# One cleared index transfer in the opening instead of six behind the first block, and GpSimd's first loop batch written out

## The chip, the cores and the metric

The kernel runs on one core of a Trainium2 chip. The metric is the device time of one execution in microseconds, median of the runs. TensorE (PE in the profile) multiplies matrices, VectorE (DVE) and ScalarE (ACT) work on rows of elements, GpSimd (POOL) does element work too and is the engine that issues the indirect transfers (gathers and scatters by a list of indices), and SyncE (SP) issues the plain transfers. Each engine runs its own instruction list in order. They meet only through semaphores: an instruction may raise one when it ends, and a later one on any engine may wait for a value.

## The reference: what is computed

Three layers in a row. The first is a linear attention over 4 batches, 8 heads, 768 steps, 48 dimensions:

```
for t in range(S):
    cur = einsum('bhd,bhe->bhde', u * k[t], v[t])
    y[t] = einsum('bhd,bhde->bhe', r[t], state + cur)
    state = w * state + einsum('bhd,bhe->bhde', k[t], v[t])
```

The second takes the 3072 rows of 384 values: `h = max(x@w1, x@w2, x@w3)` with 768 columns, then `h @ w_out`. The third is a mixture of 8 experts. Gate logits with a noise term choose the two best experts of each token, `relu(x @ w1[e]) @ w2[e]` is computed for the tokens of each expert, and the two results of a token are added with softmax weights.

## The kernel before

The attention goes in 24 chunks of 128 tokens, three of them to a block of 384 tokens, so there are 8 blocks. A block's chunks are computed while TensorE does the second layer of the block before: `period(i, b, half, attends, routes)` is one such stretch on each engine. In it TensorE does six groups of the second layer (`hidden`, three banks of PSUM each), puts the attention's products between them, and ends with three products by `w_out` (`x_product`, one for every 128 tokens). Each float32 product is made of three passes with split operands (lines 1445 to 1447, `three_pass`). Period 0 is written out on all engines, periods 1 to 6 are in a loop (`Fori(1, BATCH)`, two periods to a turn), and period 7 has no attention.

From period 1 on, each period also routes the block before it (`routes`): VectorE finds the two best experts of each token and the place of each token in its expert's list. GpSimd then writes six groups of 128 entries into `lists` in DRAM, by indirect transfers whose indices are in `row_i` (`put_entries`, L504: three groups of tokens, two choices each). An index above the bound writes nothing. The lists lie one period behind: in period i, GpSimd writes what VectorE prepared in period i-1 and completed at its end. So in period 1 there is nothing to write yet. GpSimd sets `entry` to 0 and all of `row_i` to SKIP (65535, above the bound) in the opening (L543, L544), and `put_entries(0)` in period 1 issues six transfers that write nothing but raise `listed` by 16 each. Those counts serve VectorE: `route_ranks(j)` waits until the entries that it is about to overwrite have been sent (`listed`), at 96 for the first block, at 96 more for each next one. SyncE and ScalarE wait for counts of the same semaphore near the end of the routing.

What the change and the prediction touch on the other engines: TensorE's `outputs` of the last chunk of a period (L1428, L1432) raises `y_mm`; VectorE waits for it before it adds `y_n` (L724, L726); TensorE's `turn_y` (L1440) waits for `y_n`; SyncE's load of the next values (L332) waits for `y_mm` too. At the end of period 0 this stands on TensorE as: `x_product(0, 0)`, `turn_y` of two chunks, `outputs` of chunk 5, `x_product(0, 1)`, `turn_y` of chunk 5, `x_product(0, 2)`, then period 1. ScalarE copies each `x_product` out of PSUM (`x_out`, L1225) and each turned y (L1163), and VectorE takes the low part of it (L732). The opening before period 0 has the same chain on chunk 2: `outputs`, `y_n`, `turn_y`, and then the small products `fold` (L1516).

Of the kernel before, what the change touches and what calls it, by code (L numbers as in the profile page):

```python
# [28 lines left out]
BATCH, HEADS, SEQ, HD = 4, 8, 768, 48  # L29
# [9 lines left out]
NTOK = BATCH * SEQ  # L39
# [5 lines left out]
BS = BT // P  # L45
NBLK = NTOK // BT
NE = 8
# [44 lines left out]
def build(nc, rT, kT, kN, vN, wcol, ucol, moe_w, gates, noise, ew1, ew2, out):  # L92
    ctx = ExitStack()
    with ctx:
        def sb(name, shape, dt=F32, where=None):
            return (where or ctx).enter_context(nc.sbuf_tensor(name, shape, dt))

        def sem(name):
            return ctx.enter_context(nc.semaphore(name))
# [3 lines left out]
        lists, blank = all_lists[0:NE * NTOK, :], all_lists[NE * NTOK:NE * NTOK + P, :]  # L103
# [79 lines left out]
        entry = sb("entry", [P, BS, 2, 4], I32, where=turn3)  # L183
        entry_f = sb("entry_f", [P, BS, 2, 4], where=turn3)
        row_f = sb("row_f", [P, BS, 2], where=turn3)
        row_i = sb("row_i", [P, 2, BS], I32, where=turn3)
# [57 lines left out]
        b_init = sem("b_init")  # L244
# [11 lines left out]
        entry_ok = sem("entry_ok")  # L256
        listed = sem("listed")
# [19 lines left out]
        block = ctx.enter_context(nc.Block())  # L277
        HALF = (slice(0, HB), slice(HB, P))

        def known(n, least):  # L280

            return isinstance(n, int) and n < least
# [10 lines left out]
        def _(sp):  # L293
# [99 lines left out]
            for q in range(NPE):  # L393
                if q == 3:
                    sp.wait_ge(ewh_ok, 1)
                    sp.wait_ge(ewl_ok, 1)
                src, at = (ew1, q * PIECE) if q * PIECE < W1P else (ew2, q * PIECE - W1P)
                sp.dma_start(e0_raw[q % 3][:, :], src[0, :, at:at + PIECE]).then_inc(e0_in[q % 3], 16)
                if q == 2:
                    sp.wait_ge(listed, 16 * 2 * BS * (NBLK - 1))  # L400
                    sp.wait_ge(x_stored, 16 * (NBLK - 2))
                    sp.wait_ge(x_clear, 16)
                    sp.dma_start(ent_e[:, :, :], lists[0:EARLY * ET, :].rearrange("(s p) w -> p s w", p=P)).then_inc(early_in, 16)
# [12 lines left out]
            sp.wait_ge(tile0_ok, 1)  # L416
            where = place(0, tile_0)
            sp.wait_ge(x_stored, 16 * NBLK)
            sp.wait_ge(listed, 16 * 2 * BS * (NBLK + 1))
            sp.wait_ge(xg_in, 32 * EARLY)  # L420
            load_entries(where, ent, entG_in)
            load_entries(where, ent3, entP_in)
# [20 lines left out]
        def _(pool):  # L443
# [35 lines left out]
            def own_values(b, cc):  # L479
                c, g = cc % BS, chunk(b, cc)  # L480
                pool.wait_ge(v_in[c], 16 * (2 * b + cc // BS + 1))
                pool.wait_ge(a_ok, g + 1)
                if not known(g, 1):
                    pool.wait_ge(yn_ok, g)
                pool.tensor_tensor(av[:, :].rearrange("j (n d) -> j n d", d=HD), v_sb[:, c, :, :].rearrange("j q (h d) -> j (q h) d", h=2),
                                   a_sb[:, :, :].rearrange("j q (h a) -> j (q h) a", a=1).to_broadcast([P, 2 * PAIRS, HD]),
                                   ALU.mult).then_inc(av_ok, 1)

            def prepare(b, cc):
                keys(b, cc)  # L490
                new_state(b, cc)

            def hidden_low(i, f):

                pool.wait_ge(hh_ok, F1T * i + f + 1)
                pool.tensor_tensor(hl[:, f, :], hmax[f % 3][:, :], hh[:, f, :].bitcast(F32), ALU.subtract).then_inc(hl_ok, 1)  # L496


            def put_entries(n, tokens=range(BS)):
                pool.wait_ge(entry_ok, n + 1)  # L500
                pool.sem_inc(passed, 1)
                for s in tokens:
                    for c in range(2):
                        pool.indirect_dma_start(  # L504
                            lists, bass.IndirectOffsetOnAxis(row_i[:, c, s:s + 1], 0),
                            entry[:, s, c, :], None, bounds_check=NE * NTOK - 1, oob_is_err=False).then_inc(listed, 16)

            def period(i, b, half, attends, routes):
                at = half * BS
                if attends:  # L510
                    prepare(b, at)
                if routes:
                    put_entries(i - 1)
                hidden_low(i, 0)
                hidden_low(i, 1)
                if attends:
                    own_values(b, at)
                    prepare(b, at + 1)
                hidden_low(i, 2)
                hidden_low(i, 3)  # L520
                if attends:
                    own_values(b, at + 1)
                    prepare(b, at + 2)
                hidden_low(i, 4)
                hidden_low(i, 5)
                if attends:
                    own_values(b, at + 2)
# [12 lines left out]
            pool.memset(empty[:, :, 0:1], 0).then_inc(b_init, 1)  # L540
            pool.memset(empty[:, :, 1:3], SKIP).then_inc(b_init, 1)
            pool.memset(empty[:, :, 3:4], 0).then_inc(b_init, 1)
            pool.memset(entry[:, :, :, :], 0).then_inc(b_init, 1)  # L543
            pool.memset(row_i[:, :, :], SKIP).then_inc(entry_ok, 1)  # L544
            pool.memset(pick[:, :, :, :], 0.0).then_inc(b_init, 1)
            pool.memset(zrow[:, :], 0.0).then_inc(b_init, 1)
# [2 lines left out]
            pool.iota(tok_id[:, :], [[P, BS]], base=0, channel_multiplier=1, allow_small_or_imprecise_dtypes=True).then_inc(const_ok, 1)  # L549
            pool.memset(carry[:, :], 0.0).then_inc(const_ok, 1)  # L550
            pool.iota(tile_f[:, 0, :], [[1, NTILE]], base=0, channel_multiplier=0, allow_small_or_imprecise_dtypes=True).then_inc(const_ok, 1)
            period(0, 0, 1, True, False)

            pool.wait_ge(lists_clear, 32)
            with pool.Fori(1, BATCH) as b:
                for half in range(2):
                    period(2 * b - 1 + half, b, half, True, True)

# [73 lines left out]
        def _(dve):  # L632
# [16 lines left out]
            for l in range(LEVELS):  # L649
                n = 1 << l  # L650
# [157 lines left out]
            def route_ranks(j, own, bank=7):  # L808

                rank = ps[bank][:, 0:BS * NE].rearrange("p (s e) -> p s e", s=BS)  # L810
                total = ps[bank][:, BS * NE:2 * BS * NE].rearrange("p (s e) -> p s e", s=BS)
                dve.wait_ge(rank_mm, j + 1)

                dve.wait_ge(listed, 16 * 2 * BS * (j + 1))
                for s in range(BS):
                    own(dve.tensor_tensor(POS[:, s, :], rank[:, s, :], carry[:, :], ALU.add))
                    own(dve.tensor_tensor(carry[:, :], carry[:, :], total[:, s, :], ALU.add))
                    own.settle()
                dve.sem_inc(rank_ok, 1)
# [42 lines left out]
            def period(i, b, half, attends, routes, first=False, final=False):  # L862
# [57 lines left out]
                if routes:  # L920
                    route_ranks(i - 1, own, 5 if final else 7)
# [227 lines left out]
        def _(act):  # L1149
# [43 lines left out]
            def hidden(i, f):  # L1193
                n = F1T * i + f

                act.wait_ge(h_mm, 3 * n + 1)
                if not known(n, 3):
                    act.wait_ge(hl_ok, n - 2)
                act.activation(hmax[f % 3][:, :], ps[0][:, 0:BT], ACT.Copy).then_inc(h0_ok, 1)

                act.wait_ge(hmax_ok, 2 * n + 2)
                if f == 0 and not known(i, 1):
                    act.wait_ge(x_mm, BS * i)
                act.activation(hh[:, f, :], hmax[f % 3][:, :], ACT.Copy).then_inc(hh_ok, 1)  # L1204
# [41 lines left out]
            def period(i, b, half, attends, routes, first=False, final=False):  # L1246
                at = half * BS
                for f in range(F1T):
                    hidden(i, f)
                    if attends and f in (0, 2, 4):  # L1250
                        fade(b, at + f // 2)
                    if routes and f == 0:
                        logs(i - 1)
                    if routes and f == 3:
                        gaps(i - 1)
                    if first and f < 3:
                        split_piece_high(3 + f)
                    if first and f == 1:
                        keep_gates()
                    if first and f == 2:  # L1260
                        split_fold_high(0)
                        split_fold_high(1)
                    if first and f in (3, 4):
                        split_wo_high(f - 3)
                    if final and f < NPE:
                        act.wait_ge(e0_in[f % 3], 16 * (f // 3 + 1))
                        split_high(0, f, 1, e0_raw[f % 3], f * PIECE)
                x_out(i, 0)
                if attends:
                    split_y_high(b, at, 3)  # L1270
                    split_y_high(b, at + 1, 4)
                x_out(i, 1)
                if attends:
                    split_y_high(b, at + 2, 7)
                if final:
                    turn_early(0)
                x_out(i, 2)
# [93 lines left out]
                early_high(1, q)  # L1371

            turn_rows(2)
            act.wait_ge(listed, 16 * 2 * BS * (NBLK + 1))
            act.wait_ge(plan_ok, 1)
            with act.Fori(0, NE // 2 - 1) as m:
                for par in range(2):
# [364 lines left out]
```

## Time and profile before

| | us |
|---|---|
| median of three runs (889.55 to 891.22) | 889.93 |
| the profiled execution's own time | 886.54 |
| its span, first to last instruction | 884.5 |
| TensorE busy | 869.8 |
| VectorE busy | 452.1 |
| GpSimd busy | 389.4 |
| ScalarE busy | 272.6 |

The span is what the trace covers; the execution's own time has 2.0 us around it. The runs that were timed took 3.4 us more than the profiled execution. TensorE is busy for 98% of the span, so the time is a sum of its work, of the few places where it waits and of those where its granted clock is below 1.00.

### The profile page before, as it was taken

The numbers are of one execution on the slowest core, as the hardware profiler recorded it, in microseconds if no ns is written. First come the engines' busy times: TensorE is split into PE (matmuls) and PEld (weight loads), VectorE is DVE, ScalarE is ACT, GpSimd is POOL, SyncE is SP. The second block draws the span as 40 slices with busy tenths as digits, with TensorE's granted clock in tenths as the row PEclk, the third lists the DMA queues.
The fourth block names the chain that finished last, engine by engine and source line by source line (L and its number), as shares of the span: only waits on it lengthen the run. The fifth ranks groups of instructions, "written<-read, shape, count | busy, mean of one in ns | idle before, by whom it ended". The sixth has DMA issues, their size and how long they took to land.

```text
span 884.5 us, 19490 instructions
## 1 busy us (share of the span) xinstructions
PE 869.8 (98%) x6540; PEld 846.3 (96%) x6541; DVE 452.1 (51%) x1100; ACT 272.6 (31%) x522; POOL 389.4 (44%) x380
## 2 busy tenths in 40 slices
PE   7999999999999999999999999999999999999997
PEld 5898999999999999999989999999999999999997
DVE  8762646547464655637473564353535435264322
ACT  4531323223141322225413343331414223143211
POOL 6344335344352534234443655453634435355543
PEclk9999999999999999999999999999999999999999
DMA  8894112222221221032115532624426252452222
GB/s 210 192 303 122 47 50 56 69 62 54 59 61 47 65 55 37 2 133 56 47 46 189 162 91 49 191 61 122 136 56 193 70 186 78 116 157 61 72 61 69
DMA packets 103763, 86.05 MB, mean 97 GB/s; under 512 B 60634, under 2 KB 93090, under 8 KB 103696
## 3 DMA queue, kind: packets, MB, share of 16 engines
q1 hardware_dynamic: 83152, 31.75, 15.2%
q0 software_dynamic: 12416, 26.28, 9.7%
q10 hardware_dynamic: 8128, 27.13, 9.4%
q8 instruction: 40, 0.66, 0.3%
q14 instruction: 27, 0.22, 0.1%
HBM read 70.46 MB, written 21.35 MB: 104 GB/s over the span
## 4 chain that ended last, share of the span: by engine, by line
PE 96%; issue 1%; POOL 1%; DVE 1%; another core or an unknown queue 1%; DMA 0%; ACT 0%; POOLq 0%; SPq 0%; DVEq 0%
PE ps L1445 28%; PE ps L1446 28%; PE ps L1447 28%; PE ps L1393 3%; PE ps L1432 2%; PE ps L1497 2%; PE ps L1428 2%; PE ps L1404 2%; PE ps L1419 1%; PE ps L1440 1%; POOL k_hat L466 1%; PE ps L1516 0%; DVE tables L652 0%; PE ps L1509 0%
## 5 line engine op out<-in xcount | busy, mean ns | idle before, releaser
L1445 PE MATMUL ps<-yh,wh 128*128 128x384 f32 x432 | 147.6, 342 | 0.7 <-ACT x_sb L1225 0.7
L1336 ACT ACTIVATE gh<-ps 128x384 fp32r<-128x384 f32 x136 | 67.0, 493 | 262.1 <-PE ps L1447 242.6
L1446 PE MATMUL ps<-xgl,w1h 128*128 128x384 f32 (+1 forms) x456 | 145.7, 320 | 1.5 <-issue 1.3
L1445 PE MATMUL ps<-xgh,w1h 128*128 128x384 f32 (+1 forms) x456 | 145.8, 320 | 0.5 <-issue 0.5
L1447 PE MATMUL ps<-xgh,w1l 128*128 128x384 f32 (+1 forms) x456 | 145.6, 319 | 0.3 <-issue 0.3
L1447 PE MATMUL ps<-yh,wl 128*128 128x384 f32 x432 | 144.6, 335 | 0.0
L1446 PE MATMUL ps<-yl,wh 128*128 128x384 f32 x432 | 144.5, 334 | 0.0
L1085 DVE SCALAR_TENSOR_TENSOR gl<-ps,gh 128x384 fp32r<-128x384 f32 x136 | 75.9, 558 | 129.6 <-ACT gh L1336 118.3
L1445 PE MATMUL ps<-w2h,gh 128*128 128x384 f32 x408 | 138.1, 338 | 0.0
L1446 PE MATMUL ps<-w2l,gh 128*128 128x384 f32 x408 | 136.5, 335 | 0.0
L1447 PE MATMUL ps<-w2h,gl 128*128 128x384 f32 x408 | 136.5, 335 | 0.0
L496 POOL TENSOR_TENSOR hl<-hmax,hh 128x384 fp32r<-128x384 f32 x48 | 51.5, 1073 | 129.6 <-ACT hh L1204 129.6
L590 POOL DMA_INDIRECT xg<-x_rows,ent x57 | 67.6, 1186 | 79.5 <-DMA ent<-lists 32.5
L760 DVE TENSOR_TENSOR hmax<-hmax,ps 128x384 f32<-128x384 f32 x96 | 53.2, 554 | 84.3 <-PE ps L1447 59.1
L504 POOL DMA_INDIRECT lists<-entry,row_i x54 | 54.0, 1000 | 85.1 <-DVEq L860 71.2
L617 POOL DMA_INDIRECT out<-yrow,ent x51 | 58.7, 1151 | 70.3 <-DVE yrow L1106 60.5
L1447 PEld LDWEIGHTS ps<-xgh,w1l 128*128 128x128 f32 x456 | 86.9, 191 | 1.6 <-issue 1.6
L1445 PEld LDWEIGHTS ps<-xgh,w1h 128*128 128x128 f32 x456 | 86.8, 190 | 1.2 <-issue 1.1
L1446 PEld LDWEIGHTS ps<-xgl,w1h 128*128 128x128 f32 x456 | 86.9, 191 | 0.3 <-issue 0.3
L1445 PEld LDWEIGHTS ps<-yh,wh 128*128 128x128 f32 x432 | 81.1, 188 | 3.0 <-issue 1.2
L608 POOL DMA_INDIRECT prev<-out,ent x51 | 52.1, 1022 | 70.0 <-issue 69.7
L1446 PEld LDWEIGHTS ps<-yl,wh 128*128 128x128 f32 x432 | 81.2, 188 | 0.0
(205 smaller groups left out, 1519.8 us busy)
## 6 DMA issues: line engine op xcount, KB each, us to landing
ew_raw<-ew ACTq DMA_DIRECT2D x28, 768.0 KB
v_sb<-vN SPq DMA_DIRECT2D x24, 192.0 KB, 2.7
out<-zrow SPq DMA_DIRECT2D x1, 4608.0 KB, 15.2
x_rows<-x_sb ACTq DMA_DIRECT2D x8, 576.0 KB
kn_sb<-kN SPq DMA_DIRECT2D x20, 192.0 KB, 3.6
k_raw<-kT SPq DMA_DIRECT2D x48, 72.0 KB, 1.9
wraw<-moe_w SPq DMA_DIRECT2D x6, 576.0 KB, 7.9
r_raw<-rT SPq DMA_DIRECT2D x44, 72.0 KB, 2.0
```

Source lines behind the costliest of these rows:

```text
L496: pool.tensor_tensor(hl[:, f, :], hmax[f % 3][:, :], hh[:, f, :].bitcast(F32), ALU.subtract).then_inc(hl_ok, 1)
L504: pool.indirect_dma_start(lists, bass.IndirectOffsetOnAxis(row_i[:, c, s:s + 1], 0), entry[:, s, c, :], None, bounds_check=NE * NTOK - 1, ...
L590: pool.indirect_dma_start(xg[:, s, :], None, x_rows, bass.IndirectOffsetOnAxis(ent[:, s, 0:1], 0), bounds_check=FAR, oob_is_err=False).the ...
L608: pool.indirect_dma_start(prev[:, s, :], None, out, bass.IndirectOffsetOnAxis(ent3[:, s, 2:3], 0), bounds_check=FAR, oob_is_err=False).the ...
L617: pool.indirect_dma_start(out, bass.IndirectOffsetOnAxis(ent2[:, s, 1:2], 0), yrow[:, s, :], None, bounds_check=FAR, oob_is_err=False).the ...
L760: dve.tensor_tensor(hmax[f % 3][:, :], hmax[f % 3][:, :], ps[1 + j][:, 0:BT], ALU.max).then_inc(hmax_ok, 1)
L1085: dve.scalar_tensor_tensor(gl[:, f, :], ps[f % 4][:, 0:T], 0.0, gh[:, f, :].bitcast(F32), ALU.max, ALU.subtract).then_inc(gl_ok, 1)
L1336: act.activation(gh[:, f, :], ps[f % 4][:, 0:T], ACT.Relu).then_inc(gh_ok, 1)
L1393: mm = pe.matmul(ps[bank + h][:, p * CH:(p + 1) * CH], k_hat[cc % 2][rows, p, :], q_hat[cc % 2][rows, p, :], start=True, stop=True)
L1445: pe.matmul(o, ah, bh, start=start, stop=False)
L1446: pe.matmul(o, ah, bl, start=False, stop=False)
L1447: return pe.matmul(o, al, bh, start=False, stop=stop)
```

## The change

A helper gives the count of `listed` after the entries of n blocks: `sets_put(n)` is 16 (one transfer in the opening) and 96 for each block. All waits for `listed` go by it. `entry` is cleared in one group only, and the opening ends with one indirect transfer of it with SKIP indices. Period 1 has `routes` False on GpSimd, so it issues no transfer. Periods 1 and 2 are written out ahead of the loop, which now starts at 2, and the wait for the cleared lists stands behind period 1. On the other engines only the values of the waits differ.

```diff
--- before.py
+++ after.py
@@ -277,6 +277,10 @@
         block = ctx.enter_context(nc.Block())
         HALF = (slice(0, HB), slice(HB, P))
 
+        def sets_put(n):
+
+            return 16 * (1 + 2 * BS * n)
+
         def known(n, least):
 
             return isinstance(n, int) and n < least
@@ -397,7 +401,7 @@
                 src, at = (ew1, q * PIECE) if q * PIECE < W1P else (ew2, q * PIECE - W1P)
                 sp.dma_start(e0_raw[q % 3][:, :], src[0, :, at:at + PIECE]).then_inc(e0_in[q % 3], 16)
                 if q == 2:
-                    sp.wait_ge(listed, 16 * 2 * BS * (NBLK - 1))
+                    sp.wait_ge(listed, sets_put(NBLK - 2))
                     sp.wait_ge(x_stored, 16 * (NBLK - 2))
                     sp.wait_ge(x_clear, 16)
                     sp.dma_start(ent_e[:, :, :], lists[0:EARLY * ET, :].rearrange("(s p) w -> p s w", p=P)).then_inc(early_in, 16)
@@ -416,7 +420,7 @@
             sp.wait_ge(tile0_ok, 1)
             where = place(0, tile_0)
             sp.wait_ge(x_stored, 16 * NBLK)
-            sp.wait_ge(listed, 16 * 2 * BS * (NBLK + 1))
+            sp.wait_ge(listed, sets_put(NBLK))
             sp.wait_ge(xg_in, 32 * EARLY)
             load_entries(where, ent, entG_in)
             load_entries(where, ent3, entP_in)
@@ -540,7 +544,7 @@
             pool.memset(empty[:, :, 0:1], 0).then_inc(b_init, 1)
             pool.memset(empty[:, :, 1:3], SKIP).then_inc(b_init, 1)
             pool.memset(empty[:, :, 3:4], 0).then_inc(b_init, 1)
-            pool.memset(entry[:, :, :, :], 0).then_inc(b_init, 1)
+            pool.memset(entry[:, 0, 0, :], 0).then_inc(b_init, 1)
             pool.memset(row_i[:, :, :], SKIP).then_inc(entry_ok, 1)
             pool.memset(pick[:, :, :, :], 0.0).then_inc(b_init, 1)
             pool.memset(zrow[:, :], 0.0).then_inc(b_init, 1)
@@ -549,10 +553,15 @@
             pool.iota(tok_id[:, :], [[P, BS]], base=0, channel_multiplier=1, allow_small_or_imprecise_dtypes=True).then_inc(const_ok, 1)
             pool.memset(carry[:, :], 0.0).then_inc(const_ok, 1)
             pool.iota(tile_f[:, 0, :], [[1, NTILE]], base=0, channel_multiplier=0, allow_small_or_imprecise_dtypes=True).then_inc(const_ok, 1)
+            pool.wait_ge(entry_ok, 1)
+            pool.wait_ge(b_init, 4)
+            pool.indirect_dma_start(lists, bass.IndirectOffsetOnAxis(row_i[:, 0, 0:1], 0), entry[:, 0, 0, :], None,
+                                    bounds_check=NE * NTOK - 1, oob_is_err=False).then_inc(listed, 16)
             period(0, 0, 1, True, False)
-
+            period(1, 1, 0, True, False)
             pool.wait_ge(lists_clear, 32)
-            with pool.Fori(1, BATCH) as b:
+            period(2, 1, 1, True, True)
+            with pool.Fori(2, BATCH) as b:
                 for half in range(2):
                     period(2 * b - 1 + half, b, half, True, True)
 
@@ -811,7 +820,7 @@
                 total = ps[bank][:, BS * NE:2 * BS * NE].rearrange("p (s e) -> p s e", s=BS)
                 dve.wait_ge(rank_mm, j + 1)
 
-                dve.wait_ge(listed, 16 * 2 * BS * (j + 1))
+                dve.wait_ge(listed, sets_put(j))
                 for s in range(BS):
                     own(dve.tensor_tensor(POS[:, s, :], rank[:, s, :], carry[:, :], ALU.add))
                     own(dve.tensor_tensor(carry[:, :], carry[:, :], total[:, s, :], ALU.add))
@@ -1371,7 +1380,7 @@
                 early_high(1, q)
 
             turn_rows(2)
-            act.wait_ge(listed, 16 * 2 * BS * (NBLK + 1))
+            act.wait_ge(listed, sets_put(NBLK))
             act.wait_ge(plan_ok, 1)
             with act.Fori(0, NE // 2 - 1) as m:
                 for par in range(2):
```

GpSimd's instruction list in the opening, before. The memsets and iotas end it, and the first work of period 0 follows:

```order
L549 IOTA tok_id 128x3
L550 MEMSET carry 128x8
L551 IOTA tile_f 128x26
L466 TENSOR_TENSOR k_hat<-k_raw,tables 128x512 [waits s_mm,rk_in0]
L476 TENSOR_TENSOR k_upd<-kn_sb,wu_nat 128x384 [waits u_mm,kn_in0]
```

The same place now:

```order
L553 IOTA tok_id 128x3
L554 MEMSET carry 128x8
L555 IOTA tile_f 128x26
L558 DMA lists<-entry,row_i 24576x4 [waits b_init,entry_ok]
L470 TENSOR_TENSOR k_hat<-k_raw,tables 128x512 [waits s_mm,rk_in0]
```

One indirect transfer has come between the last iota and period 0's first key product, with waits for GpSimd's own memsets.

GpSimd at the border of periods 0 and 1, before. `av` is the last work of period 0, and the loop starts at the branch:

```order
L485 TENSOR_TENSOR av<-v_sb,a_sb 128x384 [waits yn_ok,a_ok,v_in2]
L555 UNCONDITIONAL_BRANCH [waits lists_clear]
L555 ISA
L465 ISA [waits rk_in0]
L466 TENSOR_TENSOR k_hat<-k_raw,tables 128x512 [waits s_mm]
L472 REGISTER_ALU
L475 REGISTER_ALU [waits kn_in0]
L476 TENSOR_TENSOR k_upd<-kn_sb,wu_nat 128x384 [waits u_mm]
L500 REGISTER_ALU
L504 DMA lists<-entry,row_i 24576x4 [waits entry_ok]
L504 DMA lists<-entry,row_i 24576x4 x5
L495 ISA
```

The same place now:

```order
L489 TENSOR_TENSOR av<-v_sb,a_sb 128x384 [waits yn_ok,a_ok,v_in2]
L470 TENSOR_TENSOR k_hat<-k_raw,tables 128x512 [waits s_mm,rk_in0]
L480 TENSOR_TENSOR k_upd<-kn_sb,wu_nat 128x384 [waits u_mm,kn_in0]
L500 TENSOR_TENSOR hl<-hmax,hh 128x384 [waits hh_ok] x2
L489 TENSOR_TENSOR av<-v_sb,a_sb 128x384 [waits yn_ok,a_ok,v_in0]
```

The six transfers and the branch are gone from here. The branch into the loop now stands behind period 2.

## Rows read from the trace of the kernel before

**Rows 1.** The page: span and busy time of each engine.
```profile
span 884.5 us, 19490 instructions
PE 869.8 (98%) x6540; PEld 846.3 (96%) x6541; DVE 452.1 (51%) x1100; ACT 272.6 (31%) x522; POOL 389.4 (44%) x380
```

**Rows 2.** Waits of PE: waiter, releaser, us in total, times, longest.
```profile
PE ps L1440 <- DVE y_n L726: 2.0, 1, 2.0
```

**Rows 3.** Timeline of PE: start, us, instruction; in brackets idle time before and releaser.
```profile
73.82 0.39 PE L1432 MATMUL ps<-v_sb,scores 128*64 128x48 f32 x8
...
77.33 0.34 PE L1447 MATMUL ps<-woh,hl 128*128 128x400 f32 x1
79.64 0.52 PE L1440 MATMUL ps<-ident,y_n 128*128 128x128 f32 x3 [1.97 <-DVE y_n L726]
...
84.10 0.54 PE L1445 MATMUL ps<-woh,hh 128*128 128x400 f32 x1
```

**Rows 4.** Timelines of DVE, SP and ACT, the same stretch.
```profile
78.87 0.46 DVE L724 TENSOR_TENSOR y_n<-ps,av 128x288 f32<-128x288 f32 x1 [5.07 <-remote]
...
78.86 0.39 SPq L332 DMA_DIRECT2D v_sb<-vN  x1
...
81.83 0.51 ACT L1225 ACTIVATE x_sb<-ps 128x400 f32<-128x400 f32 x1 [8.70 <-remote]
```

**Rows 5.** Windows: us, busy time of each engine, PEclk, DMA share, GB/s.
```profile
82.00:84.00 2.00, 2.00 (x7) 1.97 (x7) 1.25 (x3) 0.72 (x2) 0.00 (x0) 0.50 0.00 0
```

**Rows 6.** Timeline of POOL around the six transfers.
```profile
73.12 1.16 POOL L504 DMA_INDIRECT lists<-entry,row_i  x1 [0.17 <-issue]
...
79.69 0.97 POOL L504 DMA_INDIRECT lists<-entry,row_i  x1 [0.30 <-issue]
91.13 1.00 POOL L496 TENSOR_TENSOR hl<-hmax,hh 128x384 fp32r<-128x384 f32 x1 [10.46 <-ACT hh L1204]
```

**Rows 7.** Timelines around period 2's batch: POOL, then PE, then ACT, then DVE.
```profile
137.04 1.01 POOL L504 DMA_INDIRECT lists<-entry,row_i  x1 [9.08 <-DVEq L860]
...
143.48 0.97 POOL L504 DMA_INDIRECT lists<-entry,row_i  x1 [0.30 <-issue]
...
141.40 0.33 PE L1447 MATMUL ps<-yh,wl 128*128 128x384 f32 x1
...
145.68 0.49 ACT L1199 ACTIVATE hmax<-ps 128x384 f32<-128x384 f32 x1 [1.54 <-PE ps L1447]
...
140.30 0.56 DVE L760 TENSOR_TENSOR hmax<-hmax,ps 128x384 f32<-128x384 f32 x1 [1.10 <-issue]
```

**Rows 8.** Period 1's end: `outputs` in the chain, `y_n` in DVE's timeline.
```profile
128.22 0.22 PE ps L1432 x8
...
128.49 0.46 DVE L724 TENSOR_TENSOR y_n<-ps,av 128x288 f32<-128x288 f32 x1
```

**Rows 9.** The chain: third attention products of a period, first ones of the next.
```profile
66.89 1.09 PE ps L1393 x16
94.39 1.09 PE ps L1393 x16
...
274.52 1.09 PE ps L1393 x16
298.50 1.09 PE ps L1393 x16
```

**Rows 10.** The opening: timelines of POOL, DVE and PE.
```profile
31.54 1.38 POOL L466 TENSOR_TENSOR k_hat<-k_raw,tables 128x512 f32<-128x512 f32 x1 [6.28 <-DMA r_raw<-rT]
...
26.46 0.46 DVE L724 TENSOR_TENSOR y_n<-ps,av 128x288 f32<-128x288 f32 x1 [0.56 <-PE ps L1432]
26.84 0.25 DVE L726 TENSOR_TENSOR y_n<-ps,av 128x96 f32<-128x96 f32 x1
...
27.57 0.55 PE L1440 MATMUL ps<-ident,y_n 128*128 128x128 f32 x3
```

**Rows 11.** DMA queues in 74 to 76 us: packets, MB, share.
```profile
q8 instruction: 1, 0.02, 4.4%
```

## The prediction

> **What bounds the kernel now.** I read the page first. TensorE is busy 869.8 of 884.5 us, over 98% [rows 1]. So an edit on GpSimd is worth only what it changes in TensorE's idle time or clock. The list of TensorE's waits is the next view. Past the start its longest entry is 2.0 us, once, at L1440 behind VectorE's y_n [rows 2]. That one is to be followed, because it stands beside the six transfers that the change takes away.
>
> The timeline of TensorE shows it. `outputs` of chunk 5 ends at 73.82 + 0.39 = 74.21, `x_product(0, 1)` ends at 77.67, and then TensorE stands until 79.64 because `turn_y` needs y_n [rows 3]. VectorE began that y_n at 78.87, after 5.07 us idle, though its inputs were long made: the product ended at 74.21, 4.66 us earlier. The profile puts the wait down to "remote", that is, to nothing it knows. SyncE's load of values, which waits for the same semaphore, starts at 78.86. ScalarE's copy of `x_product(0, 1)` starts at 81.83, 4.16 us after that product's end [rows 4]. Three engines that wait for a signal of TensorE all got it over 4 us late. At the end of period 1 the same y_n starts at 128.49, 0.05 us behind its product [rows 8].
>
> What lies beside it is GpSimd's batch: six transfers from 73.12 to 80.66, 0.97 us each and 0.30 between them [rows 6]. The last late signal comes 81.83 - 80.66 = 1.17 us behind the last transfer. Period 2's batch has the same mark: its last transfer ends at 144.45, TensorE's first-bank product (L1447) ends at 141.73, and ScalarE, waiting for it at the end, starts at 145.68, which is 1.23 us behind the batch [rows 7]. There TensorE does not stop, since nothing it needs soon hangs on that signal. So I read it thus: while GpSimd issues a batch of indirect transfers, TensorE's signals can reach the others some 4 us late, and only at the end of period 0 does TensorE itself need the answer at once.
>
> The stand has a sequel. In 82 to 84 us the granted clock is 0.50, the lower of its two levels (1.2 GHz), and the matmul at 84.10 takes 0.54 us where the one at 77.33 takes 0.34 [rows 3, 5]. TensorE had stood for 1.97 us shortly before the fall.
>
> **The change part by part.** *Six transfers leave period 1.* GpSimd gets 7.54 us back (73.12 to 80.66), none of it on the path: its next work waited for ScalarE until 91.13 anyway, 10.46 us of idle [rows 6]. What counts is the late signal. With no batch there, I take y_mm to arrive at 74.2 as in period 1. Then y_n is done by 75.0, 2.7 us before TensorE asks for it, so the 1.97 us go, and with them the fall of the clock. The size is taken from the chain instead of from those two pieces: from the third attention products of period 0 to the first ones of period 1 is 94.39 - 66.89 = 27.50 us. The same stretch between periods 4 and 5, with the same instructions on TensorE and no wait, is 298.50 - 274.52 = 23.98 [rows 9]. The difference is 3.52 us. The pieces agree: 1.97 of it is the stand, and the 1.55 left are what some 3.1 us at half the clock lose, of which the 2 us of [rows 5] are a part. What is late next is nothing: that other stretch has no stop at all.
>
> *One transfer enters the opening.* It starts where GpSimd fell idle, at 31.54 - 6.28 = 25.26, and the engine has nothing else to do until 31.54, when its data arrives [rows 10]. Its 0.97 to 1.16 us [rows 6] are hidden five times over in the 6.28 us of idle. Queued behind it is only that key product. But its mark on TensorE's signals has to be bounded. In the opening the chain is tight: y_mm for chunk 2 gives y_n at 26.46, done at 27.09, and TensorE starts `turn_y` at 27.57 without a wait [rows 10], so the slack is 0.48 us. From below: no delay, as at first in period 2's batch, which began at 137.04: VectorE's L760, which waits for TensorE, had its signal by 140.30 [rows 7]. The cost is 0. By the mark of the batches: the transfer ends at about 25.3 + 1.16 = 26.46, release comes 1.17 us later, at 27.63, y_n starts 1.17 us late, and beyond the slack TensorE loses 0.7 us. From above: the longest delay seen, 4.66 us, less the slack, 4.2 us. I take 0.4, between the first two, since a single transfer is nearest to the start of a batch.
>
> *The count waits.* `route_ranks(0)` waits for 16 in place of 96 and finds it long reached. Later waits are for the same transfers as before, each count being 80 lower. *Written-out periods 1 and 2.* The same work on GpSimd without register arithmetic; a code block more or less to load is hidden in idle stretches like the 10.46 us before 91.13. The wait for the cleared lists moves behind period 1, over 50 us after it was met. *The smaller memset* is 0.12 us on an idle engine. Each of these is 0.
>
> **Sum.** -3.5 + 0.4 = -3.1 us. On the profiled execution that is 886.54 - 3.1 = 883.4. The timed runs are at 889.93, 3.4 above it, and I carry the same difference over: 889.93 - 3.1 = 886.8 us.
>
> The Trainium skill has a rule against this reading. The page "SBUF — State Buffer", section "Who interferes with whom", says that transfers never contend with a compute engine, and that TensorE and ScalarE wait for no one. By that rule the batch couldn't have held TensorE up and the sum would be 0 (889.9 us). The trace agrees that TensorE's own reads went on, since the matmuls run on through the batch; that its signals came 4 us late is in rows 4, and the rule says nothing of signals.
>
> **The rivals.** *A: the late signal has another cause, and it stays.* One candidate is loading of code: TensorE comes to its loop here, and in 74 to 76 us one packet of code was loaded [rows 11]. The others are the many loads that SyncE issues at this time, and the profiler itself, in which case the timed runs never had the stand. For it: period 2's late signal cost nothing, so there is one costly case only. Against it: both late cases lie by a batch and end 1.2 us behind it, and TensorE's instructions did go on through 74 to 77.67. The time is then that of before, 889.9 us, or 890.3 with the opening's 0.4. The page "Runtime: NRT & Kernel Launch", section "Instruction fetch mechanics", states that a taken branch out of the loaded window stalls for a fetch; by that rule the stand would belong to the loop and the time would be the 889.9 of this rival.
>
> *B: slower, the delay moves into the opening.* There SyncE's loads are dense too. The point that decides is y_mm of chunk 2: each microsecond that it is held beyond 0.48 is one that TensorE stands. If it is held as long as at 74.21, that is 4.2 us of stand, and a stand of that length brings the half clock with it, 1.5 us as above: 5.7 - 3.5 = +2.2, 892.1 us. It breaks even at a delay of 2.5 us with a fall of the clock (2.0 + 1.5). Against it: one transfer instead of six, ended before the late part of any batch seen.
>
> *C: half of it.* The stand is shorter but not gone, because VectorE or ScalarE is late for its own reasons, and the clock still falls: -1.6 us, 888.3.
>
> **How the numbers follow.** My forecast has 0.68, A 0.18, B 0.07, C 0.07. About 0.2% (1.8 us) is what a measurement of this kernel can tell from no change. The forecast lies at 886.4 (nothing lost in the opening) to 887.1 (0.7 lost), and with the spread of the runs (0.4 below and 1.3 above their median) at 885.5 to 888.1. It gives nearly all of "faster", 0.70 with a share of C; "same" has A and most of C, 0.22; "slower" is B, 0.08. For the range I reach from 885.4 over C and A to 890.5, which leaves out B and the tails.
>
> **What would show it.** Right: TensorE's 2.0 us behind y_n (L726 before, L735 now) is gone from the list of waits; y_n of chunk 5 starts near 74.3 and has no "remote" before it; the granted clock is 1.00 in 82 to 84; the stretch between the products is near 24.0 us; in the opening y_n starts by 27.6. Wrong: y_n stays late with no transfer of GpSimd near it (A), or TensorE stands at the `turn_y` of 27.57 (B), or the profile shows the gain and the timed runs don't (A, the profiler).

## The result and the profile after

The changed kernel takes 883.77 us (median of 6 runs, 882.47 to 885.45), and the kernel before 890.39 (6 runs of the same comparison, 889.02 to 891.48). The ratio is 0.9925, its interval 0.9913 to 0.9937, so the change saves 6.6 us. I had forecast 886.8, some 3.1 saved. The direction was right, the size half of what came, and the time lies below my range.

The profiled execution of the changed kernel took 883.59 us. This is its page.

```profile
span 881.8 us, 19454 instructions
PE   867.1 (98%) x6540; PEld 844.5 (96%) x6541; DVE 451.3 (51%) x1100; ACT 272.1 (31%) x522; POOL 383.4 (43%) x375
```

TensorE is busy 2.7 us less than in [rows 1] with the same 6540 instructions: part of its work ran at a higher clock. GpSimd has five instructions fewer. TensorE's list of waits (columns as in [rows 2]) begins so:

```profile
PE ps L1582 <- POOLq L462: 4.1, 1, 4.1
PE ps L1402 <- POOL k_hat L470: 1.8, 2, 1.1
PE ps L1456 <- issue: 1.5, 2, 1.0
PE ps L1455 <- issue: 1.0, 1, 1.0
PE ps L1454 <- ACT x_sb L1234: 0.7, 1, 0.7
```

The 2.0 us behind y_n of [rows 2] are gone, and no entry of this list stands in that stretch: the first is at the program's start, the waits for `k_hat` are at 10 and 16 us, the others behind 180 us. The timelines of VectorE, ScalarE and GpSimd answer to [rows 4] and [rows 6]:

```profile
74.29 0.46 DVE L733 TENSOR_TENSOR y_n<-ps,av 128x288 f32<-128x288 f32 x1 [0.45 <-PE ps L1441]
...
77.75 0.50 ACT L1234 ACTIVATE x_sb<-ps 128x400 f32<-128x400 f32 x1 [4.58 <-PE ps L1456]
...
87.39 1.01 POOL L500 TENSOR_TENSOR hl<-hmax,hh 128x384 fp32r<-128x384 f32 x1 [14.41 <-ACT hh L1213]
```

y_n starts at 74.29, where [rows 4] had 78.87, and ScalarE copies `x_product(0, 1)` at 77.75 in place of 81.83. Both have TensorE as their releaser again, not "remote". The windows (columns as in [rows 5]) and the chain of the stretch of [rows 9] show what TensorE makes of it:

```profile
80.00:84.00 4.00, 4.00 (x25) 4.00 (x24) 0.87 (x4) 0.99 (x2) 0.00 (x0) 1.00 0.49 158
```

```profile
66.93 1.09 PE ps L1402 x16
90.66 1.09 PE ps L1402 x16
```

The clock stays at 1.00, and the stretch takes 90.66 - 66.93 = 23.73 us, where [rows 9] had 27.50. In the opening, timelines of GpSimd, VectorE and TensorE answer to [rows 10]:

```profile
25.45 1.50 POOL L558 DMA_INDIRECT lists<-entry,row_i  x1 [0.19 <-issue]
...
26.93 0.46 DVE L733 TENSOR_TENSOR y_n<-ps,av 128x288 f32<-128x288 f32 x1 [1.00 <-PE ps L1441]
...
27.61 0.55 PE L1449 MATMUL ps<-ident,y_n 128*128 128x128 f32 x3
```

y_n starts 0.47 us later than before, at the very end of the transfer (25.45 + 1.50 = 26.95). It stays within the slack: TensorE has `turn_y` at 27.61, against 27.57.

The two profiled executions differ by 886.54 - 883.59 = 2.95 us, close to my sum of 3.1, but by luck: the stretch alone gave 27.50 - 23.73 = 3.77, the opening cost next to nothing, and about 1 us of the lead was lost again in small pieces behind the stretch (3.7 us at 90.66, 2.7 between the spans). The timed runs differ by 6.6. That was the riddle the experiments had to solve.

### The profile page after: what moved, and what is told of

The parts are those of the page before. It is cut to its first block, busy times and chain, and to the rows that moved or that the text cites. A ratio compares the mean times of both kernels' runs of the same rounds, so it can differ in the third digit from the quotient of the medians.

```text
span 881.8 us, 19454 instructions
## 1 busy us (share of the span) xinstructions
PE 867.1 (98%) x6540; PEld 844.5 (96%) x6541; DVE 451.3 (51%) x1100; ACT 272.1 (31%) x522; POOL 383.4 (43%) x375
## 4 chain that ended last, share of the span: by engine, by line
PE 97%; issue 1%; POOL 1%; DVE 1%; DMA 0%; POOLq 0%; ACT 0%; SPq 0%; DVEq 0%
PE ps L1454 28%; PE ps L1455 28%; PE ps L1456 28%; PE ps L1402 3%; PE ps L1441 2%; PE ps L1506 2%; PE ps L1437 2%; PE ps L1413 2%; PE ps L1428 1%; PE ps L1449 1%; POOL k_hat L470 1%; PE ps L1525 0%; DVE tables L661 0%; DMA u_sb<-ucol 0%; PE ps L1518 0%
## 5 line engine op out<-in xcount | busy, mean ns | idle before, releaser
L1454 PEld LDWEIGHTS ps<-yh,wh 128*128 128x128 f32 x432 | 81.1, 188 | 3.2 <-issue 1.4
L508 POOL DMA_INDIRECT lists<-entry,row_i x48 | 47.2, 983 | 83.4 <-DVEq L869 71.2
```

What stands on the lines that cost most here:

```text
L508: pool.indirect_dma_start(lists, bass.IndirectOffsetOnAxis(row_i[:, c, s:s + 1], 0), entry[:, s, c, :], None, bounds_check=NE * NTOK - 1, ...
L1454: pe.matmul(o, ah, bh, start=start, stop=False)
```

## The experiments

My theory at this point: GpSimd's batch of indirect transfers delays TensorE's signals, and taking it away is the whole gain. Rival: the written-out periods, the code that they load or the loads of SyncE are behind the delay. The first four kernels ran on one chip, with 23 runs of the kernel before, median 890.12 (886.26 to 891.75).

**The kernel before, profiled again.** No edit.

> The kernel before, unchanged, run again for its spread and for a second trace. Theory 1 (the late signal at the end of period 0 costs more in a typical execution than in the one first traced): y_n of chunk 5 again starts over 4 us behind its product, and the stretch between the third attention products of period 0 and the first of period 1 is 27.5 us or more, up to 30.6, since the timed runs lost 6.6 us against the changed kernel and the two traces 2.7. Theory 2 (the first trace was simply a fast execution, and a typical one has more stops or half-clock stretches elsewhere): that stretch is again about 27.5 us, and some 3 us more are lost behind it, most likely at 435 to 460 us.

Measured: 889.97 us (12 runs, 887.96 to 892.25), ratio 1.0 (0.9987 to 1.0012). Its profiled execution took 890.85, 4.3 us more than the one I had predicted from. The same stretch of it, in TensorE's waits, then in the timelines of VectorE and GpSimd:

```profile
PE ps L1440 <- DVE y_n L726: 4.9, 1, 4.9
```

```profile
81.59 0.46 DVE L724 TENSOR_TENSOR y_n<-ps,av 128x288 f32<-128x288 f32 x1 [8.01 <-remote]
...
72.90 1.16 POOL L504 DMA_INDIRECT lists<-entry,row_i  x1 [0.18 <-issue]
...
79.47 0.97 POOL L504 DMA_INDIRECT lists<-entry,row_i  x1 [0.30 <-issue]
```

The product behind which y_n waits ended at 73.61 + 0.39 = 74.00, so the signal was 7.6 us late instead of 4.7. TensorE stood 4.9 us instead of 2.0. Here y_n too had to wait out the whole batch: it starts 1.15 us behind the batch's end (79.47 + 0.97 = 80.44), which is the mark that ScalarE alone had in [rows 4, 6]. The windows (columns as in [rows 5]) and the chain, with its own entry for the delay:

```profile
80.00:84.00 4.00, 1.64 (x6) 1.66 (x7) 0.83 (x3) 0.99 (x2) 0.45 (x1) 0.52 0.20 49
84.00:88.00 4.00, 4.00 (x16) 3.97 (x16) 2.00 (x6) 0.00 (x0) 0.00 (x0) 0.63 0.05 15
```

```profile
66.68 1.09 PE ps L1393 x16
...
73.59 7.99 another core or an unknown queue
...
97.65 1.09 PE ps L1393 x16
```

The stretch takes 97.65 - 66.68 = 30.97 us. Against 23.73 that is 7.24 us: 4.91 of stand, and the other 2.3 from the low clock. TensorE's timeline has the clock at its lower level (1.2 GHz; a 400-column product takes 0.54 us instead of 0.34) until 87.0. Taken off this execution, 890.85 - 7.24 = 883.61, which is the time of the changed kernel's first profiled execution (883.59); that it agrees so closely is partly chance, since the second one, below, took 882.29 with the same stretch.

**The changed kernel again.** No edit.

> The changed kernel, unchanged, run again. Both theories: the stretch is 23.7 to 24.0 us, and no wait of TensorE for y_n. It should be 6 to 7 us faster than the kernel before, as in the timed runs (ratio about 0.9925).

Measured: 883.73 us (881.8 to 884.58), ratio 0.9927 (0.9915 to 0.9939). The stretch is 23.73 us, the same as in the first trace. So it took 27.50 and 30.97 us in two executions with the six transfers in it, and the same time in two without them.

**Periods 1 and 2 written out, the six transfers kept.**

```diff
-            with pool.Fori(1, BATCH) as b:
+            for half in range(2):
+                period(1 + half, 1, half, True, True)
+            with pool.Fori(2, BATCH) as b:
```

> The kernel before with only the other part of the change: periods 1 and 2 are written out on GpSimd, the six transfers stay where they were. If the six transfers are the cause of the late signal: as slow as before (within 0.2%), y_n again over 4 us late. If it was loading of code or the branch into GpSimd's loop: as fast as the changed kernel, -6 us.

Measured: 890.02 us (12 runs, 888.3 to 892.12), ratio 1.0 (0.9989 to 1.0011). TensorE's waits and VectorE's timeline:

```profile
PE ps L1442 <- DVE y_n L728: 4.8, 1, 4.8
```

```profile
81.95 0.46 DVE L726 TENSOR_TENSOR y_n<-ps,av 128x288 f32<-128x288 f32 x1 [7.95 <-remote]
```

The chain of the stretch:

```profile
67.10 1.09 PE ps L1395 x16
...
97.84 1.09 PE ps L1395 x16
```

The stretch takes 30.74 us, in an execution (889.92) that lies at the median of its kernel, so the long delay is likely the usual one, and the 27.50 of the first trace a mild case. Writing the periods out gives nothing, and the delay is not GpSimd's branch or what it loads. TensorE's own entry into its loop, with the packet of code in 74 to 76 us, is not tested by this edit, but the changed kernel has both (one packet in 74 to 76 us there too) and no delay.

**One transfer at the old place, none in the opening.** The changed kernel, with period 1 routing again but with five of its six transfers skipped.

```diff
+                        if known(n, 1) and (s or c):
+                            continue
...
-            pool.indirect_dma_start(lists, bass.IndirectOffsetOnAxis(row_i[:, 0, 0:1], 0), entry[:, 0, 0, :], None,
-                                    bounds_check=NE * NTOK - 1, oob_is_err=False).then_inc(listed, 16)
             period(0, 0, 1, True, False)
-            period(1, 1, 0, True, False)
+            period(1, 1, 0, True, True)
```

> The changed kernel with its one transfer at the old place of the six (behind k_upd in period 1) and none in the opening. If a batch must last some us before TensorE's signals come late: no delay, as fast as the changed kernel. If any transfer beside SyncE's loads delays them until 1.2 us behind its end: the transfer would end at about 74.3, the signal due at 74.2 comes at 75.5, y_n is done by 76.2, ahead of the 77.7 where TensorE asks for it, so again no loss of time but a visible delay of 1.3 us. If the length of the batch does not matter: y_n 4 us late and the time of the kernel before.

Measured: 884.34 us (883.88 to 884.86), ratio 0.9933 (0.992 to 0.9946). Timelines of GpSimd and VectorE:

```profile
72.90 1.16 POOL L510 DMA_INDIRECT lists<-entry,row_i  x1 [0.17 <-issue]
...
74.45 0.46 DVE L731 TENSOR_TENSOR y_n<-ps,av 128x288 f32<-128x288 f32 x1 [0.87 <-PE ps L1439]
```

The transfer ends at 74.06 and the product at 73.99. y_n is 0.46 us late, about as in the changed kernel's opening, and TensorE has no wait. A transfer at the old place does no harm while it is alone; the 0.6 us between this median and that of the changed kernel (883.73) lie within the spread of the runs. The next four kernels ran beside 14 runs of before, median 890.66 (888.53 to 892.99).

**Six transfers in the opening, none in period 1.** A direct test of rival B. The counts of `listed` and the clearing of `entry` follow, here and in the kernel with three transfers.

```diff
-            pool.indirect_dma_start(lists, bass.IndirectOffsetOnAxis(row_i[:, 0, 0:1], 0), entry[:, 0, 0, :], None,
-                                    bounds_check=NE * NTOK - 1, oob_is_err=False).then_inc(listed, 16)
+            for s in range(BS):
+                for c in range(2):
+                    pool.indirect_dma_start(lists, bass.IndirectOffsetOnAxis(row_i[:, c, s:s + 1], 0), entry[:, s, c, :], None,
+                                            bounds_check=NE * NTOK - 1, oob_is_err=False).then_inc(listed, 16)
```

> The changed kernel with six transfers in the opening in place of one (rival B's case on purpose). They take about 25.4 to 33.0 us. Theory 1 (a batch holds TensorE's signals while it runs, until about 1.2 us behind its end): y_mm of chunk 2, due at 26.4, comes as late as 34, TensorE stands some 6 us at turn_y, and with the half clock behind it the kernel is 6 to 9 us slower than the changed one, so as slow as before or slower. Theory 2 (only the end of period 0 is sensitive, by its own loads or TensorE's entry into its loop): the opening is not delayed and the time is that of the changed kernel, 884.

Measured: 884.52 us (884.39 to 884.55), ratio 0.9924 (0.9896 to 0.9952). Timelines of GpSimd and VectorE:

```profile
25.48 1.49 POOL L560 DMA_INDIRECT lists<-entry,row_i  x1 [0.18 <-issue]
...
33.01 0.97 POOL L560 DMA_INDIRECT lists<-entry,row_i  x1 [0.30 <-issue]
...
26.96 0.46 DVE L735 TENSOR_TENSOR y_n<-ps,av 128x288 f32<-128x288 f32 x1 [1.03 <-PE ps L1443]
```

The batch of six runs from 25.48 to 33.98, yet y_n starts at the end of the first transfer (26.97) and not of the last. The same coincidence, within 0.06 us, is in all six traces that I compared with a transfer here. Rival B falls. So does my reading that a batch holds TensorE's signals to its end wherever it stands.

**SyncE's loads held back.** The kernel before, with the ten loads of one chunk, which SyncE issued at 72.7 to 78.9 us, waiting until the six transfers have landed. To do it, the first turn of SyncE's loop is written out, which wasn't run by itself.

```diff
-            with sp.Fori(1, BATCH) as b:
+            for cc in range(2 * BS):
+                if cc == 2:
+                    sp.wait_ge(listed, 16 * 2 * BS)
+                load_turned(1, cc)
+                load_keys(1, cc)
+                load_values(1, cc)
+            with sp.Fori(2, BATCH) as b:
```

> The kernel before with its six transfers where they were, but SyncE's ten loads of chunk (1, 2), which it issued at 72 to 79 us beside them, wait until all six have landed. Theory S (the signals are late only where SyncE issues loads beside the batch): y_n of chunk 5 starts at 74.3 and the time is that of the changed kernel, -6 us. Theory G (GpSimd's batch alone does it): y_n as late as before, 79 to 82, and the time of the kernel before.

Measured: 886.22 us (10 runs, 885.17 to 888.63), ratio 0.9955 (0.994 to 0.9971). TensorE's waits and VectorE's timeline:

```profile
PE ps L1446 <- DVE y_n L732: 1.2, 1, 1.2
```

```profile
77.81 0.46 DVE L730 TENSOR_TENSOR y_n<-ps,av 128x288 f32<-128x288 f32 x1 [4.35 <-remote]
...
81.48 0.51 ACT L1231 ACTIVATE x_sb<-ps 128x400 f32<-128x400 f32 x1 [8.68 <-remote]
```

The batch ends at 80.32, but the signal for y_n comes 3.9 us late, before its end. ScalarE's, for a product that ended at 77.33, still comes 4.1 us late and 1.16 us behind the batch, with no load issued between 71 and 81.4 us. So the batch delays signals without the loads too. TensorE stands twice, 1.24 us for y_n and 0.85 behind ScalarE's late copy, and the clock stays at 1.00 through both. The edit saves 4.4 of the 6.6 us or so. The outcome lies between the theories: in the timed runs less is lost without the loads, but the delay doesn't go.

**Three transfers at the old place.** As the kernel with one, but `s * 2 + c >= 3` is the test for skipping.

```diff
+                        if known(n, 1) and s * 2 + c >= 3:
+                            continue
```

> Three transfers at the old place in period 1, none in the opening. They end at about 72.9 + 3.7 = 76.6. If the signals are held until 1.2 us behind the batch: y_n starts at 77.8, done at 78.4, and TensorE, which asks for it at 77.5, stands about 1 us; the kernel is 1 to 2 us slower than the changed one. If the delay is there as soon as there are two or more and has its own length: y_n at 79 or later and the time of before. If it needs more than three: no delay.

Measured: 885.56 us (882.7 to 885.78), ratio 0.9934 (0.9912 to 0.9956). TensorE's waits, then GpSimd's last transfer and y_n:

```profile
PE ps L1447 <- DVE y_n L733: 0.6, 1, 0.6
```

```profile
75.77 0.97 POOL L510 DMA_INDIRECT lists<-entry,row_i  x1 [0.30 <-issue]
...
77.42 0.46 DVE L731 TENSOR_TENSOR y_n<-ps,av 128x288 f32<-128x288 f32 x1 [3.71 <-remote]
```

y_n starts 0.68 us behind the shorter batch (76.74). The release follows the batch's end. This trace is of the fastest execution, 2.9 us below the median, so the usual delay of this kernel may be longer than the one shown.

**Six transfers, with a pause behind the second.** The kernel with the periods written out, and one wait of GpSimd for the y_n in question:

```diff
                 for s in tokens:
+                    if known(n, 1) and s == 1:
+                        pool.wait_ge(yn_ok, 2 * BS)
                     for c in range(2):
```

> Six transfers in period 1, periods 1 and 2 written out, and one wait added on GpSimd: behind the second transfer it waits until VectorE has made y_n of chunk 5. If the signals come through as soon as GpSimd pauses: the second transfer ends at about 75.3, y_n starts at about 76.5 and is done at 77.1, just before TensorE asks for it, and the kernel is as fast as the changed one, with all six transfers still there. If their number or what they leave in the queues makes the delay: y_n at 79 or later.

Measured: 883.68 us (882.38 to 884.38), ratio 0.9915 (0.9885 to 0.9945). GpSimd and VectorE:

```profile
74.52 0.97 POOL L506 DMA_INDIRECT lists<-entry,row_i  x1 [0.30 <-issue]
77.45 0.97 POOL L506 DMA_INDIRECT lists<-entry,row_i  x1 [1.97 <-DVE y_n L730]
...
76.04 0.46 DVE L728 TENSOR_TENSOR y_n<-ps,av 128x288 f32<-128x288 f32 x1 [2.31 <-remote]
...
77.64 0.50 ACT L1229 ACTIVATE x_sb<-ps 128x400 f32<-128x400 f32 x1 [4.58 <-PE ps L1451]
81.23 0.50 ACT L1229 ACTIVATE x_sb<-ps 128x400 f32<-128x400 f32 x1 [2.70 <-PE ps L1451]
```

This settles where the cost comes from. All six transfers are issued in period 1 and the whole gain of the change is there. The signal comes 1.9 us late, 0.55 us after GpSimd pauses (75.49), and TensorE loses nothing. But the row of four behind the pause, from 77.45 to 82.36, didn't hold up ScalarE's signals: its two copies start 0.04 us behind the ends of their products (77.60 and 81.19). So not every row of transfers delays a signal in period 1 either, and what decides it is open.

**The same thing elsewhere.** In the changed kernel TensorE stops several times at 449 to 453 us (in the kernel before at 454 to 456), late in the first expert's work, where six transfers into the lists and two scatters stand in a row on GpSimd. Three kernels ran together beside 11 runs of before, median 887.98 (885.68 to 890.62): the changed one; one with a wait for ScalarE's `gh` ahead of the scatters; one with the scatters moved behind the gathers that follow.

```diff
             pool.wait_ge(out_clear, 16)
+            pool.wait_ge(gh_ok, F2T + 4)
             scatter_early(0)
```

```diff
             pool.wait_ge(out_clear, 16)
-            scatter_early(0)
...
             gather_rows(0)
+            scatter_early(0)
```

> The changed kernel again, to stand beside the next two: about 884 us, with TensorE's stops of 1.5 to 2.5 us in all at 450 to 453 us behind GpSimd's batch of eight (441 to 451), and in some executions a half-clock stretch behind them.

> The changed kernel with one wait more on GpSimd: between the six transfers of the last block's entries and the two scatters of the first early group it waits until ScalarE has taken two pairs of the second early group's products. If the same mechanism (signals of TensorE come through when GpSimd pauses) makes the late signals at 448 to 453: ScalarE's activation starts at about 449.5 in place of 453, the stops at 450 to 453 shrink from some 2 us to under 0.5, and the kernel is 1.5 to 3 us faster than the changed one. If not: no change, or slower by what the scatters are late.

> The changed kernel with the two scatters of the first early group moved behind the next gather, so that the batch is six and not eight transfers. ScalarE's activation should start at about 450 in place of 453. But VectorE waits for these scatters before its row at about 461, and they would now land at 462 or later: so a gain of up to 2 us from the stops, less about 1 us, -1 us in all, and no gain if the gather and the scatters make one long batch of five again.

Measured: 881.9 us (880.54 to 883.07) for the changed kernel, ratio 0.9932 (0.9914 to 0.9951); 880.34 (879.78 to 880.76) with the wait, ratio 0.9915 (0.9898 to 0.9932); 880.53 (880.05 to 881.24) with the scatters later, ratio 0.9918 (0.9901 to 0.9935). In the changed kernel, GpSimd, ScalarE and TensorE:

```profile
450.25 0.98 POOL L577 DMA_INDIRECT out<-yrow,ent_e  x1 [0.30 <-issue]
...
452.77 1.77 ACT L1341 ACTIVATE gh<-ps 128x512 fp32r<-128x512 f32 x3 [15.68 <-remote]
...
452.62 0.28 PE L1454 MATMUL ps<-xgh,w1h 128*128 128x256 f32 x1 [1.03 <-issue]
```

With the wait, GpSimd and ScalarE:

```profile
447.25 0.97 POOL L508 DMA_INDIRECT lists<-entry,row_i  x1 [0.30 <-issue]
451.49 1.02 POOL L577 DMA_INDIRECT out<-yrow,ent_e  x1 [3.27 <-issue]
...
449.54 1.09 ACT L1342 ACTIVATE gh<-ps 128x512 fp32r<-128x512 f32 x2 [12.78 <-PE ps L1457]
```

ScalarE starts 1.54 us behind the batch of eight (451.23) without a pause, and at 449.54, 1.3 us behind the sixth transfer (448.22), with one. Four stops of TensorE, 2.2 us in sum, are gone between 449 and 453, and two of 0.19 and 0.73 us are new at 453 and 455. That leaves 1.3 us of the 1.56 that the medians differ by. Both edits save some 1.5 us beside the changed kernel of the same comparison, and the kernel with the wait, at 880.34 us, beats both kernels. Its runs overlap with those of the changed kernel at one end (880.76 against 880.54), and the medians lie 1.56 us apart. The kernel with the scatters later overlaps more (881.24 against 880.54), so its 1.4 us are less sure.

## Why the prediction was right and wrong, by its steps

- *What bounds the kernel, and what delays y_n*: right. TensorE's 2.0 us behind y_n came from signals held during GpSimd's batch. Three edits of the batch alone (one transfer, three, a pause) move the delay; writing the periods out doesn't. It was too broad all the same: a batch in the opening holds a signal only to the end of its first transfer, and the row of four behind the pause holds none.
- *Six transfers leave, -3.5*: this is the step that failed, by its size. In the pair of profiled executions it came out nearly as computed, 3.77 (27.50 - 23.73). In the two other traces with an unbroken batch and all loads the term is about twice that: 7.24 in the second trace of before (4.9 of stand and 2.3 of low clock, against my 1.97 and 1.55), and 7.01 with the periods written out. That the timed runs, which have no trace, lose as much is inferred from their difference of 6.6. I had sized the delay from one execution, in which y_n got through ahead of the batch's end, and that execution was a mild one.
- *Carrying the difference over, 889.93 - 3.1*: wrong for the same reason, and the numbers shown would have told. The profiled execution of before stood 3.4 us below the median and 3.0 below the lowest of its three timed runs. I took that as a constant offset. It was in the main the shorter delay itself: the execution with the stretch of 30.74, 3.24 us longer, took 889.92, and the changed kernel's profiled execution, 883.59, has no such offset to its median of 883.77. Other profiled executions lie off their medians too, by up to 2.9 us, so this is no rule. Of the 23 runs of before beside the first experiments one (886.26) was as fast.
- *One transfer in the opening, +0.4*: the delay exists and is smaller than I had put it, 0.45 to 0.5 us. The slack of 0.48 takes it: `turn_y` starts 0.04 us later, and no more of a cost is to be seen. My end of 0.7 assumed the 1.17 us that follow a long batch, and it put the transfer's end at 26.46, where it was 26.95 (the transfer took 1.50 us, not 1.16).
- *Count waits, written-out periods, smaller memset, 0 each*: right. The written-out periods with six transfers have a ratio of 1.0. The other two have no trace of a cost and weren't run by themselves.
- *The spread*: from 886.4 to 887.1 with 0.4 below and 1.3 above the forecast would reach from 886.0 to 888.4, not from 885.5 to 888.1. The measured 883.77 lies below either.
- *Rival A*: falls for code loading (GpSimd's by the run with written-out periods; TensorE's because the changed kernel loads its packet too, without a delay) and for the profiler (the timed runs gain more than the profiled ones). Of SyncE's loads a part may be true: with one chunk of them held back 4.4 us are saved and the delay is 3.9 us, though that edit also writes out a turn of SyncE's loop. Without a batch they delay nothing: the changed kernel has them all.
- *Rival B*: falls. Even with six transfers in the opening the time is 884.52, and its interval overlaps that of the change. *Rival C*: no, nothing of the stand or of the low clock is left.

The Trainium skill's rule that I had weighed ("SBUF — State Buffer", section "Who interferes with whom": TensorE and ScalarE wait for no one) would have made the sum 0. By it the kernel with the pause should have gained nothing, and it gained 7 us. The rule may hold for the data ports it speaks of; of signals between engines it says nothing, and these traces have them up to 7.6 us late.

## What to carry to other kernels

Where an engine waits for a long-finished TensorE product and the profile names no releaser, look at what GpSimd does: a row of indirect transfers can hold the signal until it pauses, so try a short wait in the row where TensorE needs an answer soon, and measure it, since not every row held a signal here. Whether other work in place of the wait does the same wasn't tried. An indirect transfer that writes nothing (all its indices out of bounds) takes GpSimd as long as one that writes, 0.97 us in period 1 as in period 2. And before a stall is priced from one profiled execution, compare that execution's own time with the spread of the timed runs: if it lies outside, the stall, too, may have another size there, and the price should be a range over executions and not one number.

## What the runs showed of the hardware that I had not expected

- A signal of TensorE can reach the other engines 4.7 to 7.6 us late during six indirect transfers of GpSimd in a row (3.9 with SyncE's loads held back), 3.3 during three, 1.9 with a pause behind the second, 0.46 with one. It arrives 0.4 to 1.5 us after GpSimd pauses, except where it gets through earlier, as y_n did in the first trace (78.87, with the batch's end at 80.66). In a row of four behind a pause two signals were not late at all. What holds a signal isn't shown.
- The length of the delay changes between executions of the same kernel at the same place (4.7 and 7.6 us). Why is open; SyncE's loads may play a part.
- In the opening the signal passes behind the first transfer of six. Why it does there and not in period 1 is open.
- A stand can cost more than its length, which a list of waits doesn't show. TensorE stood 1.97 us, and its granted clock was 0.50 from about 81.1 to 84.6, some 3.4 us of work and 1.8 us lost (3.77 - 1.97). It stood 4.91, and the clock was 0.50 from 80.2 to 87.0; the first 2.2 us of that were still the stand, so it worked at half speed for 4.6 us and lost 2.3. Behind stands of 0.60 and 1.24 us the clock stayed at 1.00.
- Whether a row of other GpSimd work with as few gaps would hold signals too wasn't tried.
